# Last token tile's v product with high and low parts side by side, and the first four spatial groups in another order, in a fused attention and gated-MLP kernel

## What is computed

```
h = np.maximum(x @ w_in, 0.0)                 # x: 576 x 512, w_in: 512 x 1024
u, v = (h[..., :d_ff // 2], h[..., d_ff // 2:])
v_n = (v - mean(v)) / np.sqrt(var(v) + 1e-06) # per token, over 512 columns
v_s = np.einsum('ts,bsd->btd', w_spatial, v_n) + b_spatial[None, :, None]
gated = u * v_s
return (gated @ w_out)
```

## Time and profile before

| | |
|---|---|
| median of 3 runs | 610.12 us (610.01 to 611.67) |
| the profiled execution: its own time | 609.56 us |
| its span, first to last instruction | 607.8 us |
| mean granted TensorE clock | 0.992 of full speed |
| matmuls | 4416 |

### The profile page before, as it was taken

How to read it: one execution, slowest core, us unless ns; L and a number is a source line. 1 busy time by engine, 2 the same in 40 slices (tenths; PEclk the granted TensorE clock), 3 DMA queues, 4 the chain that set the end, 5 groups by cost and what they waited for, 6 DMA issues and landing times.

```text
span 607.8 us, 12100 instructions
## 1 busy us (share of the span) xinstructions
PE 561.7 (92%) x4416; PEld 481.7 (79%) x4416; DVE 368.6 (61%) x1243; ACT 333.4 (55%) x975; POOL 260.4 (43%) x445
## 2 busy tenths in 40 slices
PE   3797989998999989999999999999999999999895
PEld 1576978598877779999787778999787678999784
DVE  4996452257778873246778873236777884336773
ACT  2876432145668683334768773234767864324662
POOL 5765313024525752243534653252633664151521
PEclk9998999999999999999999999999999999999997
DMA  8900821000000033020000015020000000000001
GB/s 233 262 2 23 238 70 55 25 1 1 36 28 18 2 87 71 0 79 2 23 24 36 1 43 116 1 79 0 20 27 36 2 1 1 1 1 2 1 36 44
DMA packets 29743, 26.23 MB, mean 43 GB/s; under 512 B 5810, under 2 KB 22194, under 8 KB 29684
## 3 DMA queue, kind: packets, MB, share of 16 engines
q1 hardware_dynamic: 29684, 25.46, 15.0%
HBM read 20.74 MB, written 4.72 MB: 42 GB/s over the span
## 4 chain that ended last, share of the span: by engine, by line
PE 75%; DVE 11%; POOL 5%; issue 4%; ACT 3%; DMA 1%; SPq 1%; DVEq 0%; POOLq 0%; ACTq 0%
PE bank L1095 16%; PE bank L1097 16%; PE bank L1096 16%; PE bank L1126 9%; PE bank L1085 9%; PE bank L1111 3%; POOL p L513 2%; DVE neg L934 2%; PE bank L1275 2%; DVE pt_lo L842 2%; PE bank L1276 2%; ACT q L672 1%; POOL ring L430 1%; DVE q L997 1%; DMA kz<-kT 1%
## 5 line engine op out<-in xcount | busy, mean ns | idle before, releaser
L1095 PE MATMUL bank<-pt_hi,vv 128*64 128x128 f32 (+1 forms) x528 | 107.5, 235 | 13.0 <-issue 8.0
L842 DVE TENSOR_TENSOR pt_lo<-bank,pt_hi 128x512 fp32r<-128x512 f32 (+5 forms) x176 | 84.2, 493 | 41.7 <-ACT pt_hi L582 40.1
L430 POOL TENSOR_SCALAR ring<-ring,r 128x256 f32<-128x256 f32 (+2 forms) x160 | 73.8, 474 | 78.9 <-DVE r L792 78.9
L1097 PE MATMUL bank<-pt_hi,vv 128*64 128x128 f32 (+1 forms) x528 | 101.4, 224 | 0.0
L1096 PE MATMUL bank<-pt_lo,vv 128*64 128x128 f32 (+1 forms) x528 | 101.3, 224 | 0.0
L582 ACT CAST pt_hi<-bank 128x512 fp32r<-128x512 f32 (+5 forms) x176 | 72.8, 432 | 51.5 <-PE bank L1126 49.8
L1095 PEld LDWEIGHTS bank<-pt_hi,vv 128*64 128x64 f32 x528 | 71.9, 136 | 27.1 <-issue 20.2
L557 ACT ACTIVATE ring<-ring,neg 128x256 f32<-128x256 f32 (+2 forms) x160 | 75.1, 473 | 16.6 <-DVE neg L780 16.2
L1085 PE MATMUL bank<-kz,q 128*128 128x512 f32 (+2 forms) x160 | 73.9, 551 | 9.6 <-DMA kz<-kT 9.6
L513 POOL TENSOR_SCALAR p<-p,r,wgt 128x128 f32<-128x128 f32 (+4 forms) x80 | 51.9, 653 | 69.9 <-DVE r L792 65.3
L1096 PEld LDWEIGHTS bank<-pt_lo,vv 128*64 128x64 f32 x528 | 72.1, 137 | 8.6 <-issue 2.9
(11 more groups left out here) (143 smaller groups left out, 1614.9 us busy)
## 6 DMA issues: line engine op xcount, KB each, us to landing
q<-qT SPq DMA_DIRECT2D x16, 256.0 KB, 4.2
kz<-kT SPq DMA_DIRECT2D x32, 128.0 KB, 4.4
v_raw<-v SPq DMA_DIRECT2D x16, 256.0 KB, 3.6
out<-o_sb SPq DMA_DIRECT2D x16, 256.0 KB, 2.0
w_in_raw<-w_in SPq DMA_DIRECT2D x2, 1024.0 KB, 7.1
w_cat_raw<-wcat SPq DMA_DIRECT2D x1, 1544.0 KB, 7.0
w_spatial_raw<-wsT SPq DMA_DIRECT2D x1, 1152.0 KB, 10.5
w_outT_raw<-woT SPq DMA_DIRECT2D x1, 1024.0 KB, 5.3
```

What stands on the lines that cost most here:

```text
L430: last = nc.gpsimd.tensor_scalar(p, p, r1[0:r, i % 2, h:h + 1], 0.0, ALU.mult, ALU.add)
L842: last = nc.vector.tensor_tensor(pt_lo[0:r, g % 2, c0:c1], bank[0:r, 2 + g % 2, c0:c1], pt_hi[0:r, g % 2, c0:c1].bitcast(F32), ALU.subtract)
L1095: nc.tensor.matmul(to, hi_l, hi_r, start=first, stop=False)
L1097: return nc.tensor.matmul(to, lo_l, hi_r, start=False, stop=last)
```

## The change

It has three parts. First, POOL gathers the high and the low part of the last tile's x side by side in a new tile `xs` (named x_last_both), as soon as the low part is there, and the last v product becomes four times `stacked`, 8 matmuls instead of 12; ACT now copies the upper half of bank 7, DVE adds the lower half, and ACT takes the relu from SBUF to SBUF. Second, u product 4 and its relu move ahead of the last v product and its relu. Third, the first four spatial groups run their 12 matmuls over the full tiles one after the other, and only then the two of the last tile for each; groups 4 to 7 are as before.

```diff
+        xs = sb("x_last_both", [P, KT, P], F32R, at + 4 * KT * S)
...
                 rstd_of(NT - 2)
+                pool.wait_ge(s1_xl, 2 * NT * (b + 1))
+                nc.gpsimd.tensor_copy(xs[:, :, 0:LAST], x_hi[:, :, S - LAST:S])
+                nc.gpsimd.tensor_copy(xs[:, :, LAST:P], x_lo[:, :, S - LAST:S]).then_inc(s1_xs, 1)
                 for i in range(NT - 3, NT - 1):
                     low_vn(i, 0)
                     low_vn(i, 1)
...
                     if i >= 2:
                         act.wait_ge(s1_vn, NT * b + i - 1)
+                    if i == NT - 1:
+                        nc.scalar.copy(v_sb[0:r, i % 2, :], bank[r:P, 7, :]).then_inc(s1_vc, 1)
+                        act.wait_ge(s1_va, b + 1)
+                        nc.scalar.activation(v_sb[0:r, i % 2, :], v_sb[0:r, i % 2, :], ACT.Relu).then_inc(s1_v, 1)
+                        return
                     nc.scalar.activation(v_sb[0:r, i % 2, :], bank[0:r, 7, :], ACT.Relu).then_inc(s1_v, 1)
...
                 high_vn(NT - 2)
+                relu_u(4)
                 relu_v(NT - 1)
-                relu_u(4)
                 relu_u(5)
...
                 norm_v(NT - 2)
+                dve.wait_ge(s1_vc, b + 1)
+                nc.vector.tensor_tensor(v_sb[0:LAST, (NT - 1) % 2, :], bank[0:LAST, 7, :], v_sb[0:LAST, (NT - 1) % 2, :],
+                                        ALU.add).then_inc(s1_va, 1)
                 stats_v(NT - 1)
...
-                    last = three(bank[0:r, 7, :], x_hi[:, k, tok(qb)], x_lo[:, k, tok(qb)],
-                                 win_hi[:, k, FF // 2:FF], win_lo[:, k, FF // 2:FF], k == 0, k == KT - 1)
+                    w_hi, w_lo = win_hi[:, k, FF // 2:FF], win_lo[:, k, FF // 2:FF]
+                    if r < P:
+                        last = stacked(bank[:, 7, :], xs[:, k, :], w_hi, w_lo, k == 0, k == KT - 1)
+                    else:
+                        last = three(bank[0:r, 7, :], x_hi[:, k, tok(qb)], x_lo[:, k, tok(qb)], w_hi, w_lo, k == 0, k == KT - 1)
...
+                    if i == 4:
+                        pe.wait_ge(s1_xl, 2 * NT * (b + 1))
...
                 u_product(3)
+                u_product(4)
                 for k in range(KT):
                     v_product(NT - 1, k)
-                for i in range(4, 8):
+                for i in range(5, 8):
                     u_product(i)
...
+                for i in range(4):
+                    spatial_full(i)
+                for i in range(4):
+                    spatial_last(i)
+                for i in range(4, 8):
+                    spatial_full(i)
+                    spatial_last(i)
```

More of the change, by code:

```diff
@@ L248, in build @@
         s1_vm, s1_v = sem("s1_v_product"), sem("s1_v_relu")
+        s1_xs, s1_vc, s1_va = sem("s1_x_last_both"), sem("s1_v_last_lo_copied"), sem("s1_v_last_added")
         s1_st, s1_mv = sem("s1_stats"), sem("s1_mean_var")
@@ L1168, in v_product @@
                     if k == 0:
-                        pe.wait_ge(s1_xl, 2 * NT * b + 2 * i + 2)
+                        if i < NT - 1:
+                            pe.wait_ge(s1_xl, 2 * NT * b + 2 * i + 2)
+                        else:
+                            pe.wait_ge(s1_xs, b + 1)
                         if i:
@@ L1207, in row, with spatial_full @@
                 u_product(3)
+                u_product(4)
                 for k in range(KT):
                     v_product(NT - 1, k)
-                for i in range(4, 8):
+                for i in range(5, 8):
                     u_product(i)
-                for i in range(8):
+                def spatial_full(i):
                     a, dt = divmod(i, 4)
@@ L1226, in row, with spatial_last @@
                               ws_hi[:, t, c], ws_lo[:, t, c], t == 0, False)
+                def spatial_last(i):
+                    a, dt = divmod(i, 4)
+                    c = slice(HALF * a, HALF * a + HALF)
                     t = NT - 1
```

## The result

| kernel | median us | lowest to highest | runs | mean granted clock of the runs |
|---|---|---|---|---|
| before | 610.12 | 608.02 to 611.67 | 7 | 0.992 in the profiled execution |
| changed | 614.35 | 611.77 to 615.08 | 7 | 0.981 to 0.989 |
| changed, run again with the experiments | 613.04 | 611.68 to 614.61 | 11 | 0.981 to 0.989 |

The ratio is 1.0063 [1.0043, 1.0084], and 1.0051 [1.0034, 1.0068] when it was run again. All 18 runs of the changed kernel together have a median near 613.1, so I take its loss as 3 to 4 us. I forecast 610.9 and a range up to 612.4; both medians of the changed kernel lie above that range.

The account below looks back on a forecast made before the run. PE's matmuls were taken to bound batches 1 to 3, the last v tile's chain batch 0. Batches 1 to 3 -2.5, batch 0 +1.7, clock +1.7 made +0.9 us; median forecast 610.9, range 608.7 to 612.4.

Parts of the forecast that it names:

- The bound, batch by batch: PE's matmuls bound batches 1 to 3; in batch 0 the last v tile's chain does, border rows queued behind it.
- Part one on PE: Last v product: 8 matmuls at 0.2325 us instead of 12, saving 0.93 us a batch, 3.72 in four.
- Part one on POOL: Two gathering copies, near 0.40 us each, hidden by u product 4: nothing taken, upper bound 0.2 us a batch.
- Rival (d): POOL's gathering late, PE waiting 1.2 us in each batch: 613.8 us, 615.5 if the clock falls too; chance 0.07.
- The chain's three steps: Last v tile: copy 0.58, sum 0.67, relu 0.61 us with handovers, where one relu of 0.59 stood: +1.3 us.
- The relu of u product 4: Batch 0, ACT: goes ahead of the last v tile's copy, up to 0.41 us long, partly overlapped, taken as 0.3.
- The third part brings nothing of its own: Spatial groups: new order avoids a 0.5 us wait for the last tile, but that is spent on the longer chain.
- its own price before group 4: Each batch: group 4 needs bank 0 free, 1.15 against 1.06 us: 0.1 us, between 0 and 0.3.
- The clock: Batch 0: PE's pause grows from 2.77 to 5.3 us, clock falls once behind it: +1.7 us, between 0.4 and 3.4.
- Rival (e): Clock stays low twice as long behind batch 0's pause: +1.7 us more, 612.6 us; chance 0.09.
- The last sum: -0.8 without the clock plus 1.7 for it, +0.9 on 609.56: 610.4 us; median forecast 610.9.

Follow-up runs that it names:

- the kernel with the chain alone: Kernel before, but in batch 0 the last v tile goes through ACT copy, DVE operation and relu from SBUF; 612.90 us, ratio 1.0041.
- filling the pause: Changed kernel plus 26 unused matmuls of 512 columns on PE in batch 0, between last u product and first spatial group; 610.15 us, ratio 0.9987.
- the third lot: Last of three lots of experiment runs, covering four kernels beside 19 runs of the kernel before, whose median was 610.04 us.
- kernel with the relus first: Changed kernel with border rows early and POOL's v tile 2 low part before gathering, relus of u products 6, 7 before last `vn_hi`; 603.62 us, 0.9887.

## Why the prediction was wrong, by its own steps

- **The bound, batch by batch: right.** PE binds batches 1 to 3 and the chain batch 0. Undoing the change in batch 0 alone turns a loss into a gain.
- **Part one on PE: right.** 0.2325 us a matmul with 128 stationary columns, 0.93 worked out and 0.93 found in the seam (from the last v product's first matmul to the spatial groups 6.66 us instead of 9.18, of which 1.59 are the u product that moved ahead). From batch to batch it is 0.84, since some 0.09 us are lost again between one seam and the next. That this matches the forecast's 0.93 - 0.1 is luck: its 0.1 stood for a wait before group 4 that didn't come. The Trainium skill, "TensorE: Matmul & The Clock Gate", section "Back-to-back issue gap", gives 216 ns for 512 columns as the gap of isolated matmuls; the traces have 0.2325 us before and after the change.
- **Part one on POOL, "I take nothing": wrong, and the step that failed.** The prediction asked only whether the copies were ready before PE (they were, in every batch). It didn't ask who works beside POOL in batch 0. There DVE's splits of `w_spatial` run just then, and the splits stretched from 2.77 to 4.26 us in front of the chain that sets the end of PE's wait. Rival (d) had POOL late for PE and not DVE slowed by POOL. The Trainium skill, "SBUF — State Buffer", section "Who interferes with whom", says that a DVE instruction with two SBUF inputs contends with a GpSimd instruction that reads SBUF. That is this case exactly: the splits read two tiles, the copies and `vn_lo` read SBUF; the traces agree, with 2.77 to 4.26 on one side and 1.43 to 2.45 on the other. A reader of the rule should have looked at 75.15 to 77.92 on DVE before moving anything there on POOL.
- **The chain's three steps: right.** +1.3 worked out, 1.38 in the trace, 1.3 in the kernel with the chain alone. The relu of u product 4 cost 0.42, where 0.3 was taken. In sum the chain is 3.2 us later where 1.6 stood, the difference being the splits.
- **The third part brings nothing of its own: right.** Alone 0.9995; within the change it is worth 0.25 us a batch, where the prediction had 0.5. In the traces its own price before group 4 was 0.02 us, not 0.1.
- **The clock: right in kind, short in size.** It was taken to fall once, for 1.7 us. Behind the pause of 6.9 us it cost 1.50 us in one trace and 2.5 in two others (a spatial stage of 16.58, 17.55 and 17.60 against 15.08), and filling the pause gave 2.9 to 4.2 us of the median back. Rival (e), the clock low twice as long, comes near at 612.6, but its chance of 0.09 left out that a longer chain makes a longer pause. Rival (d) gave 613.8, close to both medians by number alone: POOL was never late for PE.
- **The last sum.** 609.56 + 0.9 is 610.5 and the median 611.0, not 610.4 and 610.9; nothing hangs on it.

The sum with the measured terms: -2.5 for batches 1 to 3, +3.2 for batch 0's chain (the v product's 0.93 lies in front of its wait and is lost), +1.5 to 2.5 for the clock, together +2.2 to +3.2, where the forecast had -0.8 + 1.7. The medians give +3.0 over all 18 runs; by the fit above 0.7 of it is chain less v products, and 2.3 is the clock. The forecast had +0.9, so of the 2.1 us that it was short, 1.5 are the splits, put at nothing, and 0.6 the clock. The +4.2 of the first seven alone is a microsecond beyond that. Its runs had a median clock of 0.983 against 0.986 when it was run again, and 0.003 is worth just this microsecond; which pauses lowered it can't be read from one profiled execution.

## What to carry to other kernels

Before work is put on GpSimd because it has time, look at what VectorE does in that very stretch, in each batch and not only in the steady ones: a subtraction of two SBUF tiles beside it slows both, and the one on the chain passes its delay on. A saving in front of a wait is worth nothing and a longer chain behind it costs its length and then the clock, so first move what the chain doesn't need, here the border rows, out from behind it; with them moved, the kernel with the new v product gained 1.1% instead of losing 0.6%. Of that 1.1%, 0.6% is the border rows' own, and the v product adds the other 0.5%.

## What the runs showed of the hardware that was not expected

The granted clock differs from run to run of one kernel, and the time follows it. In the third lot the 19 runs of the kernel before had 607.32 us at a clock of 1.000, 608.1 at 0.997, 610.04 at 0.992 and 612.10 at 0.986: nearly 5 us with nothing changed. The kernel with the relus first ran in 600.91 at 1.000 and in 604.23 at 0.991. Pauses of 2.8 us were followed by the lower level in one profiled execution and not in two others, pauses of 4.1 us and more in each of those that were not filled. So one profiled execution can't size a clock term, and below 0.5% medians of some ten runs can mislead (1.7 us above, where 3.4 is right); runs with the same mean clock can be compared more closely.

The slowing between DVE and POOL also showed where the border rows ran beside POOL's low parts, in the kernel that moved them: the instruction at line 834 took 1.39 us where it takes 0.82 alone, and the one at line 838 0.88 instead of 0.46. The latter reads one tile only, so it isn't just subtractions of two tiles that lose time beside POOL.
